# An attention front: scores of a head pair from 64 rows each, into two PSUM banks

## What is computed

```python
# attention: B=2, H=8 heads, S=576, D=64; q, k, v are float32
scores = (1 / sqrt(D)) * q @ k.T
mask_local   = (rel >= 0) & (rel < 32)              # heads 0 to 3
mask_strided = (rel >= 0) & (pos_k % 32 == pos_q % 32)   # heads 4 to 7
scores = where(mask, scores, -1e9)
attn = exp(scores - max); attn = attn / (sum(attn) + 1e-9)
x = (attn @ v)                                      # to 1152 tokens x 512
# 8 experts, one for each token
logits = x @ w_gate + modality_bias[modality_id];  e = argmax(logits)
out1[token] = softmax(logits)[e] * (relu(x @ w1[e]) @ w2[e])
# 4 dense experts, weighted with domain_probs
out = sum_e p[:, e] * (relu(out1 @ u1[e]) @ u2[e])
```

## Time and profile before

| what | us |
|---|---|
| three timed runs | 679.78, 681.57, 681.97 |
| median of them | 681.57 |
| span of the profiled execution, first to last instruction | 679.5 |
| attention and last gate logits in it, until | 75.6 |
| from there to the end | 603.9 |
| PE busy in the whole span | 635.0 (93%) |

### The profile page before, as it was taken

How to read it: one execution, slowest core, us unless ns; L and a number is a source line. 1 busy time by engine, 2 the same in 40 slices (tenths; PEclk the granted TensorE clock), 3 DMA queues, 4 the chain that set the end, 5 groups by cost and what they waited for, 6 DMA issues and landing times.

```text
span 679.5 us, 9341 instructions
## 1 busy us (share of the span) xinstructions
PE 635.0 (93%) x3433; PEld 555.3 (82%) x3434; DVE 249.8 (37%) x472; ACT 165.2 (24%) x401; POOL 166.2 (24%) x117
## 2 busy tenths in 40 slices
PE   5979688899998994999999999999999999999997
PEld 4869676678866883899999999999999999999996
DVE  5767638642277224233222222222222222222222
ACT  3756317532266121111111111111111111111110
POOL 6433240008520003100710700800800801600000
PEclk9979799899999997899999999999999999999999
DMA  9999358881474013200030030030020110000111
GB/s 224 219 335 369 125 209 276 297 326 51 173 272 168 31 46 107 63 0 1 1 123 1 1 123 1 3 122 0 25 99 0 56 68 0 0 0 0 46 46 46
DMA packets 30990, 68.90 MB, mean 101 GB/s; under 512 B 4728, under 2 KB 7416, under 8 KB 30968
## 3 DMA queue, kind: packets, MB, share of 16 engines
q1 hardware_dynamic: 21432, 40.29, 18.5%
q0 software_dynamic: 5792, 21.50, 9.0%
q10 hardware_dynamic: 3744, 6.82, 2.8%
HBM read 51.04 MB, written 17.56 MB: 101 GB/s over the span
## 4 chain that ended last, share of the span: by engine, by line
PE 66%; issue 13%; POOL 7%; DMA 7%; SPq 3%; DVE 2%; ACT 1%; ACTq 0%; DVEq 0%; POOLq 0%
PE bank L1033 30%; PE bank L1043 29%; DMA u_raw<-in_moe_w 3%; POOL u_lo L409 3%; DMA w_raw<-in_moe_w 2%; POOL x_by_slot L391 2%; SPq L275 1%; PE bank L860 1%; PE bank L881 1%; POOL u_hi L406 1%; DMA dprob<-in_moe_domain_probs 1%; PE bank L913 1%; PE bank L974 1%; PE bank L891 1%; PE bank L855 1%
## 5 line engine op out<-in xcount | busy, mean ns | idle before, releaser
L1033 PE MATMUL bank<-x2T_hi,u_hi 128*128 128x384 f32 x384 | 129.4, 337 | 1.5 <-DVE x2T_lo L809 1.5
L1033 PE MATMUL bank<-x2T_hi,u_lo 128*128 128x384 f32 x384 | 129.2, 336 | 0.0
L1033 PE MATMUL bank<-x2T_lo,u_hi 128*128 128x384 f32 x384 | 129.2, 336 | 0.0
L541 ACT ACTIVATE h_hi<-bank 128x384 fp32r<-128x384 f32 x96 | 47.2, 492 | 332.5 <-PE bank L1033 332.5
L1043 PE MATMUL bank<-u_hi,h_lo 128*128 128x512 f32 x288 | 112.7, 391 | 0.0
L1043 PE MATMUL bank<-u_hi,h_hi 128*128 128x512 f32 x288 | 112.6, 391 | 0.0
L1043 PE MATMUL bank<-u_lo,h_hi 128*128 128x512 f32 x288 | 112.5, 391 | 0.0
L819 DVE SCALAR_TENSOR_TENSOR h_lo<-bank,h_hi 128x384 fp32r<-128x384 f32 x96 | 53.5, 557 | 155.6 <-ACT h_hi L541 155.6
L829 DVE SCALAR_TENSOR_TENSOR acc<-bank,prob,acc 128x512 f32<-128x512 f32 x72 | 50.5, 750 | 127.9 <-PE bank L1043 127.9
L406 POOL CAST u_hi<-u_raw 128x2048 fp32r<-128x2048 f32 x16 | 29.9, 1899 | 244.8 <-PE bank L1043 227.1
L1033 PEld LDWEIGHTS bank<-x2T_hi,u_hi 128*128 128x128 f32 x384 | 72.6, 189 | 2.8 <-issue 1.9
(11 more groups left out here) (157 smaller groups left out, 708.1 us busy)
## 6 DMA issues: line engine op xcount, KB each, us to landing
w_raw<-in_moe_w SPq DMA_DIRECT2D x10, 2048.0 KB, 9.7
u_raw<-in_moe_w POOLq DMA_DIRECT2D x16, 1024.0 KB, 7.4
x_by_slot<-zero_row SPq DMA_DIRECT2D x1, 4608.0 KB, 14.9
y_by_slot<-zero_row SPq DMA_DIRECT2D x1, 4608.0 KB, 27.2
x_tile<-x_by_slot ACTq DMA_DIRECT2D x13, 256.0 KB, 3.0
y_by_slot<-y_tile ACTq DMA_DIRECT2D x13, 256.0 KB, 2.0
qT<-in_qT SPq DMA_DIRECT2D x4, 576.0 KB, 9.2
kT<-in_kT SPq DMA_DIRECT2D x8, 288.0 KB, 10.7
```

The lines of the kernel that those rows point to most:

```text
L541: a.activation(h_hi[:, f, :], bank[f][:, 0:SB], ACT.Relu).then_inc(g_hi_kept, 1)
L1033: last = t_.matmul(bank[f][:, 0:SB], lhs[:, half, c, fs], rhs[:, c, tok], start=n == 1, stop=n == 3 * DC)
```

## The change

`kT` loses its `par` dimension and its zeros, with the fills on DVE and POOL. A head's product now contracts over its own 64 rows of `qT` and `kT`. Heads 0 and 2 of a step write into one bank and heads 1 and 3 into another: the scores of step i use banks 0 and 1 or banks 2 and 3 in turn, so two steps are open instead of three. The mask product is two products of half the width. The products with v have bank 6 alone, and the transposes of x use bank 7. q is scaled by 1/8 on POOL when it has come, in five pieces, of which three stand ahead of the normalisations of steps 2, 8 and 13; the mask value, the exponential's scale and the maximum follow from that, and DVE writes the negated maximum in one instruction. The loads of the first two steps' q and k (252 of 576 columns) come first, and the four small inputs come between the two batches; `small_steps` stands one iteration later.

```diff
-        kT = sb("kT", [P, B, PAIRS, 2, S], FP32, att)
+        kT = sb("kT", [P, B, PAIRS, S], FP32, att)
@@ SP
-                for par in range(2):
-                    p = slice(D * par, D * (par + 1))
-                    sp.dma_start(kT[p, b, c, par, :], kT_in[b, p, c, :]).then_inc(qk_in[b][kind], 16)
+                sp.dma_start(qT[:, b, c, cols], qT_in[b, :, c, cols]).then_inc(done, 16)
+                sp.dma_start(kT[:, b, c, cols], kT_in[b, :, c, cols]).then_inc(done, 16)
...
+            load_qk(0, 0, slice(0, QUEUED), qk_first)
             for b in range(B):
-                if b == 1:
-                    sp.wait_ge(kT_zeroed_g, 1)
...
+                if b == 0:
+                    sp.dma_start(gate[:], w_gate.rearrange("(c p) e -> p c e", p=P)).then_inc(gate_in, 16)
...
@@ POOL
-            g.memset(kT[:, 1:B], 0.0).then_inc(kT_zeroed_g, 1)
+            pool.wait_ge(qk_first, 32)
+            scale_q(0, 0, slice(0, QUEUED))
+            pool.wait_ge(qk_in[0][0], 32)
+            scale_q(0, 0, slice(QUEUED, S))
             for i in range(STEPS):
+                if i + 3 in Q_NEEDED:
+                    b, kind = Q_NEEDED[i + 3]
+                    pool.wait_ge(qk_in[b][kind], 32)
+                    scale_q(b, kind)
                 pool.wait_ge(inv_known, i + 1)
@@ DVE
-                if i == TILES:
+                if i == TILES + 1:
                     small_steps()
...
-                    w.reduce_max(row_max[0:R, s, :], src[0:R, :, 0:C], axis=AX.X).then_inc(vstep, 1)
-                    dve.wait_ge(vstep, st.next())
-                    w.tensor_scalar(neg_max[0:R, s, :], row_max[0:R, s, :], -SCALE, None, ALU.mult)\
-                     .then_inc(max_known, 1)
+                    w.reduce_max(neg_max[0:R, s, :].rearrange("p (k h) -> p k h", k=2), score_slot(i)[0:R, :, :, 0:C],
+                                 axis=AX.X, negate=True).then_inc(max_known, 1)
@@ PE
-                    if i >= 3:
-                        pe.wait_ge(exped, i - 2)
+                    if i >= 2:
+                        pe.wait_ge(exped, i - 1)
...
+                    for k in range(2):
+                        t_.matmul(scores[0:R, k, :, 0:C], ident_b[0:R, 0:R],
+                                  mask[0:R, 0:C].unsqueeze(1).to_broadcast([R, PAIR, C]), start=True, stop=True)
                     for h in range(HALF_H):
...
-                        last = t_.matmul(bank_s[0:R, h, 0:C], qT[:, b, c, q0:q0 + R], kT[:, b, c, h % 2, k0:k0 + C],
+                        d = slice(D * (h % 2), D * (h % 2 + 1))
+                        last = t_.matmul(scores[0:R, h % 2, h // 2, 0:C], qT[d, b, c, q0:q0 + R], kT[d, b, c, k0:k0 + C],
                                          start=False, stop=True, skip_group_check=True)
...
-                    if m >= 2:
-                        pe.wait_ge(att_kept, m - 1)
+                    if m >= 1:
+                        pe.wait_ge(att_kept, m)
```

More of the change, by code:

```diff
@@ L222, in moe_chain, with score_slot @@
         h_lo = sb("h_lo", [P, FH, SB], FP32R)
-        bank = [ctx.enter_context(nc.psum_tensor(f"bank{i}", [P, 512], FP32)) for i in range(8)]
+        banks = ctx.enter_context(nc.psum_tensor("banks", [P, 8 * 512], FP32))
+        bank = [banks[:, 512 * i:512 * (i + 1)] for i in range(8)]
+        by_bank = banks[:].rearrange("p (k w) -> p k w", k=8)
+        def score_slot(i):
+            k = 2 * (i % 2)
+            return by_bank[:, k:k + 2, 0:PAIR * P].rearrange("p k (h c) -> p k h c", h=PAIR)
         small_in, gate_in = sem("small_in"), sem("gate_in")
@@ L440, in keep_rows @@
                 act.wait_ge(x_flipped, t + 1)
-                a.copy(xtok[:, t, :], bank[0][:]).then_inc(x_kept_a, 1)
+                a.copy(xtok[:, t, :], bank[7][:]).then_inc(x_kept_a, 1)
             for i in range(STEPS + LAG_V):
@@ L456, in _ @@
                         act.wait_ge(prob_flipped, i - PB + 1)
+                    scores = score_slot(i)
                     for h in range(HALF_H):
-                        last = a.activation(prob[0:R, s, h, 0:C], bank[SCORE_BANKS[i % 3]][0:R, P * h:P * h + C], ACT.Exp,
-                                            bias=neg_max[0:R, s, h:h + 1], scale=SCALE,
-                                            accum_out=row_sum[0:R, s, h:h + 1])
+                        n = by_parity(h)
+                        last = a.activation(prob[0:R, s, n, 0:C], scores[0:R, h % 2, h // 2, 0:C], ACT.Exp,
+                                            bias=neg_max[0:R, s, n:n + 1], scale=1.0,
+                                            accum_out=row_sum[0:R, s, n:n + 1])
                     last.then_inc(exped, 1)
@@ L556, in _ @@
             st = Step()
-            for pairs in (slice(2, 4), slice(0, 2)):
-                for par in range(2):
-                    other = slice(D * (1 - par), D * (2 - par))
-                    w.memset(kT[other, 0, pairs, par, :], 0.0).then_inc(kT_zeroed, 1)
             def small_steps():
@@ L656, in _ @@
                         t = LOGITS_AT[m]
-                        w.tensor_tensor(logits[:, t, :], bank[6 + m % 2][:, P * 2:P * 2 + E], bias_tok[:, 0, t, :],
+                        w.tensor_tensor(logits[:, t, :], bank[6][:, P * 2:P * 2 + E], bias_tok[:, 0, t, :],
                                         ALU.add).then_inc(vstep, 1)
@@ L854, in flip_rows @@
                 for c in range(DC):
-                    last = t_.transpose(bank[0][:, P * c:P * (c + 1)], xT[:, c, P * t:P * (t + 1)], ident[:])
+                    last = t_.transpose(bank[7][:, P * c:P * (c + 1)], xT[:, c, P * t:P * (t + 1)], ident[:])
                 last.then_inc(x_flipped, 1)
@@ L890, in _ @@
                     for h in range(HALF_H):
-                        last = t_.transpose(bank[4 + m % 2][0:C, P * h:P * h + R], prob[0:R, m % PB, h, 0:C],
+                        last = t_.transpose(bank[4 + m % 2][0:C, P * h:P * h + R], prob[0:R, m % PB, by_parity(h), 0:C],
                                             ident[0:R, 0:R])
@@ L912, in _ @@
                         o = D * (h % 2)
-                        last = t_.matmul(bank[6 + m % 2][o:o + D, P * (h // 2):P * (h // 2) + R],
+                        last = t_.matmul(bank[6][o:o + D, P * (h // 2):P * (h // 2) + R],
                                          v_rows[0:C, m, h, :], probT[0:C, m % 2, h, 0:R], start=True, stop=True)
```

59 lines of the change are left out of this document (32 added, 27 removed).

## The result

| | us |
|---|---|
| changed kernel, median of four runs | 693.13 (690.94 to 693.94) |
| kernel before, same chip, median of four | 680.67 (679.34 to 681.97) |
| ratio, 95% interval | 1.018 (1.015 to 1.021): 12.2 us slower |
| profiled execution: span, before and after | 679.5, 688.9 |
| last gate logits in it, before and after | 75.6, 84.7 |

674.5 was forecast, with 680 as the upper end. The profiled execution (690.94 in all, the fastest of the four) shows the loss where the gain was expected: 9.1 us later at the end of the attention, and 604.2 us from there to the end, where it was 603.9.

A forecast was written before the change was run, and what follows sets the result against it. PE was taken to bound plain steps, with a stall on late small inputs. -0.5 - 0.7 - 7.4 - 0.6 + 1.7 = -7.5, with 0.5 taken off for the clock: -7.0, 681.57 to 674.5; eight-in-ten range 671 to 680.

The forecast's parts named there:

- Start, -0.5: First steps: earlier q and k let PE start 1.0 us earlier, mostly lost by step 5, which starts 0.5 us earlier.
- Score passes, -0.23 a step: Scores on PE: 64-row halves run side by side, saving 0.44 less 0.21 for two array changes, net 0.23 us a step.
- The two-bank ring, 1.93 to 2.02 a step: Steps 5 to 13: scores of i+2 wait for exponentials of i, holding steps to 1.93 to 2.02 us; gain about 0.7.
- The stall, -7.4: Steps 13 to 16: small inputs land earlier, so DVE's wait, the half clock and pipe refilling go, 7.4 us gained.
- rival of late data: Batch 1's q and k come late, POOL and PE stand at steps 11 and 16: about 3 us, 677.5, chance 0.13.
- Gate steps, -0.6: Steps 16 to 21: shorter score passes give 1.15 us, one bank for the products takes some back; 0.6 gained.
- Tail, +1.7: End of the attention: one bank forces two waits of about 1 us, less step 21's passes: 1.7 us lost (0.5 to 3).
- No overlap: Rival: row halves don't run side by side, so a step has 0.44 us more on PE; 680.7, chance 0.14.
- Banks don't bind: Rival: DVE and ACT keep ahead, so tail and ring cost nothing; 672, chance 0.12.
- The clock stays low: Rival: half arrays and short waits keep PE at 1.2 GHz through the attention, each step losing 1 to 2 us; 689, chance 0.06.

The follow-up runs named there:

- run without scaling: The changed kernel with q not scaled on POOL; scale back in the exponential, DVE multiplies the maximum by -1/8 in a second instruction: 684.19, ratio 1.0006.
- order-only kernel: The kernel before with only the four small inputs moved between the two batches and small_steps one iteration later: 674.44, ratio 0.987.
- run with padded k: The changed kernel without POOL's scaling of q and with row halves undone, k in two zero-padded copies again: 685.34, ratio 1.005.
- the fillers: Products of constants that nothing reads, on PE where it would wait, added to the changed kernel without POOL's scaling of q: 677.95, ratio 0.9955.

## Why the prediction was wrong

- **Start, -0.5.** Failed. q and k of the first two steps were there in time, but their scaling took 1.49 where I put 0.7, and PE began at 7.51, not at 6.6 to 7.0. Step 5's scaling took 3.13 where I put 1.4, and step 5 began at 18.83, 1.8 us later than before. The step that failed is the duration: I chose a value near the cast by the number of inputs. The estimate worked out from the Trainium skill, GPSIMD Engine Reference, Elementwise — side-by-side cycle accounting, 1.7 us, was too low as well.
- **What lies beside it.** This is the main error. I counted POOL's scaling as a cost on POOL alone and never asked what DVE does in those 3 us. The sum has no term for it, and a sign stood in the trace of the kernel before (16.01, above). The Trainium skill, SBUF — State Buffer, Who interferes with whom, has the rule, and I had not weighed it. The runs put 9.6 of the scaling's 11.8 us on it.
- **Score passes, -0.23 a step.** Right in direction, too large: a plain step went from 2.05 to 1.96, -0.09. The passes alone gave 0.24 (0.88 to 0.64), but the mask ahead of them and the transposes behind them became longer by 0.09 and 0.05. The two changes of the array cost about 0.35, not the 0.21 that I took. The one run that undoes the halves puts all of them at 3.2 us (±2.4).
- **The two-bank ring, 1.93 to 2.02 a step.** Right as a pitch: the maxima of steps 7 to 11 start 2.01 us apart in the run without scaling. But in the order-only kernel they stand 2.02 apart, and the -0.7 for steps 5 to 13 didn't come: from the maximum of step 6 to that of step 11 it is 10.3 us with the ring and the row halves, and 10.3 with neither. Two steps failed: the 2.10 that I took as their pitch before, an average from step 5 on, and PE's own 1.82, which is 1.96.
- **The stall, -7.4.** Right: 8.7 (6.6 to 10.7) by the times, 7.1 by the trace. The rival of late data is out: in the order-only run PE waits for no transfer after its start, and in the changed kernel POOL waits 1.2 us for one, once, at the start.
- **Gate steps, -0.6.** Didn't come. From the scores of step 16 to those of step 21 PE takes 13.9 us in the run without scaling, as against 13.7 before, with a wait of 0.73 for the one bank among them; in the changed kernel it is 15.3, the first 4 at half clock.
- **Tail, +1.7.** The mechanism was right, two waits of 1.11 and 1.16, its size wrong: 6.0. I priced the waits and not the half clock that goes with them. Two banks give back 4.3 of it, and the order-only kernel's tail (12.4 from the last maximum, 12.5 before) shows the rest.
- **Rivals.** No overlap: out. Banks don't bind: out. *The clock stays low*, 689 with a chance of 0.06, was nearest. It came as stretches, not throughout: 19 to 23, 47 to 53 and from 74 to the end of the attention in the changed kernel, besides the half rate of the start. I had spoken against it because no wait in my sum was over 1.4; it fell behind waits of 1.1. POOL's scaling added three, of 1.55 and twice 1.87. Behind the first and the third the clock fell, behind the second (33.92) it did not. One sum is off: without overlap the forecast would be 674.5 + 6.6 = 681.1, not 680.7.

The account, in us against the kernel before: the small inputs' place among the loads -8.7; POOL's scaling +11.8; the rest +9.1, of which the one bank in the tail with its clock 4.3, the half rate at the start 2.2, the last piece of half clock and the addition 1.4, and 1.2 not told apart. Together +12.2. The last three are no larger than the error of the runs that give them. Among the 1.2 is likely what one bank costs ahead of the tail: PE waits for it 1.15 us behind `small_steps` (at 37.49) and 0.73 at 50.66 in the run without scaling, and at neither place in the order-only kernel.

## What to carry to other kernels

Before an operation is moved to POOL, look at what DVE does in that stretch: `tensor_scalar` from SBUF to SBUF stands still until POOL's operation is over, be it on four elements; reductions, copies from PSUM and reciprocals don't. Price a wait on PE together with the half clock that may come behind it, and an earlier start with the rate at which the work then runs. And measure the parts one by one: here moving four small inputs was worth 8.7 us by itself, and the rest of the change, once its losses were mended, nothing that these runs can tell from zero.

## What the runs showed of the hardware

- A multiplication of 1152 float32 elements a partition on POOL: 3.12 us, 2.7 ns an element, three times the 0.93 of its cast. 504 elements take 1.49 us and 648 take 1.83.
- POOL needn't read for the hold. In the run with padded k, DVE's multiplication of four elements is held by POOL's zero fill, and a reduction from PSUM beside the same fill isn't. Timelines of POOL, then DVE:

```profile
5.87 3.93 POOL L390 MEMSET kT<- 128x4608 f32 x1
```

```profile
7.69 0.68 DVE L646 TENSOR_REDUCE row_max<-banks 126x4 f32<-126x504 f32 x1 [1.63 <-PE banks L903]
8.40 1.42 DVE L649 TENSOR_SCALAR neg_max<-row_max 126x4 f32<-126x4 f32 x1
```

- At the start, the column of the granted clock says 1.00 while the records last twice as long as later; the stretch in question of the run without scaling is this, with products with v of 1.11:

```profile
16.00:21.00 5.00, 4.93 (x30) 3.32 (x32) 2.56 (x9) 2.13 (x12) 1.69 (x2) 1.00 0.96 335
```

Until the column's first change, the lengths of like records tell the rate in these traces, not the column. The Trainium skill, TensorE: Matmul & The Clock Gate, What's actually happening, has the half rate as the default that activity lifts; the fillers, with which the full rate came at 7 instead of 21.1, agree.
